# Second copies of keys and queries by SyncE's DMA queue in place of VectorE casts

## The reference

```
q_pool = q.reshape(B, H, S // 2, 2, D).mean(axis=3)          # 576 queries of 64
scores = scale * q_pool @ k.T ; scores -= max(scores)         # 576 x 1152
attn   = exp(scores) / (sum(exp(scores)) + 1e-9) ; out = attn @ v
x = out laid out as 2304 tokens x 512
h = x @ w_in ; x = (h * sigmoid(h)) @ w_out                   # 512 -> 2048 -> 512
out = ((x @ w1) * (x @ w2)) @ w3 @ w_out2                     # 512 -> 1024 -> 512
```

## Time and profile before

| | |
|---|---|
| median of 3 runs | 1469.06 us |
| span of the profiled execution, first to last instruction | 1465.5 us |
| mean granted clock of TensorE | 0.995 of full speed |
| busy: PE, DVE, ACT, POOL | 92%, 55%, 48%, 30% |
| DMA, hardware queue | 33648 packets, 75.73 MB, 19.1% of 16 engines |

### The profile page before, as it was taken

How to read it: one execution, slowest core, us unless ns; L and a number is a source line. 1 busy time by engine, 2 the same in 40 slices (tenths; PEclk the granted TensorE clock), 3 DMA queues, 4 the chain that set the end, 5 groups by cost and what they waited for, 6 DMA issues and landing times.

```text
span 1465.5 us, 24978 instructions
## 1 busy us (share of the span) xinstructions
PE 1352.9 (92%) x8224; PEld 1296.8 (88%) x8224; DVE 799.6 (55%) x1340; ACT 697.3 (48%) x1266; POOL 434.8 (30%) x322
## 2 busy tenths in 40 slices
PE   6888888888888888889999999999999999999998
PEld 5887877787778787778899999999999899999998
DVE  7888888888888889888531111111114522122221
ACT  4776666666666666667742222222224422121211
POOL 4766656666655766655200000000000000000000
PEclk9999999999999999999999999999999999999999
DMA  6233323333323233320220000000104200000000
GB/s 155 73 81 81 95 64 80 81 79 81 91 68 81 68 92 81 79 72 24 61 65 8 1 1 1 1 0 0 43 0 153 92 1 22 23 22 1 21 21 22
DMA packets 33694, 76.34 MB, mean 52 GB/s; under 512 B 8944, under 2 KB 12144, under 8 KB 33648
## 3 DMA queue, kind: packets, MB, share of 16 engines
q1 hardware_dynamic: 33648, 75.73, 19.1%
HBM read 70.84 MB, written 4.79 MB: 52 GB/s over the span
## 4 chain that ended last, share of the span: by engine, by line
PE 77%; DVE 13%; issue 7%; DVEq 1%; DMA 1%; ACT 0%; SPq 0%; ACTq 0%
PE psum L907 21%; PE psum L908 20%; PE psum L909 20%; PE psum L923 5%; PE psum L924 4%; DVE mx L708 4%; PE psum L948 3%; PE psum L949 3%; DVE mneg L717 2%; DVE pL L726 2%; DVE mneg L719 2%; PE psum L932 1%; DVE kB L691 1%; DVE xT L732 1%; DVE qHs L702 1%
## 5 line engine op out<-in xcount | busy, mean ns | idle before, releaser
L708 DVE TENSOR_REDUCE mx<-psum 128x1 f32<-128x384 f32 (+1 forms) x480 | 253.1, 548 | 74.3 <-PE psum L924 73.7
L516 ACT ACTIVATE pF<-psum 128x576 f32<-128x576 f32 x288 | 187.7, 652 | 158.9 <-PE psum L949 156.8
L923 PE MATMUL psum<-kA,qHm 128*128 128x384 f32 (+1 forms) x480 | 172.4, 359 | 60.5 <-DVE mx L708 50.4
L836 DVE TENSOR_TENSOR gL<-gF,gH 128x384 fp32r<-128x384 f32 x96 | 53.6, 558 | 306.0 <-ACT gH L593 306.0
L424 POOL TENSOR_TENSOR pL<-pF,pH 128x576 fp32r<-128x576 f32 x93 | 143.0, 1538 | 216.8 <-ACT pH L522 216.7
L522 ACT CAST pH<-pF 128x576 fp32r<-128x576 f32 x288 | 194.5, 675 | 4.6
L726 DVE TENSOR_TENSOR pL<-pF,pH 128x576 fp32r<-128x576 f32 x195 | 187.6, 962 | 15.0 <-ACT pH L522 14.5
L907 PE MATMUL psum<-pH,vH 128*128 128x288 f32 x576 | 178.7, 310 | 1.5 <-DVE xT L732 0.7
L590 ACT ACTIVATE gF<-psum 128x384 f32<-128x384 f32 x96 | 47.3, 492 | 261.9 <-PE psum L909 261.9
L909 PE MATMUL psum<-pH,vL 128*128 128x288 f32 x576 | 171.0, 297 | 0.0
L908 PE MATMUL psum<-pL,vH 128*128 128x288 f32 x576 | 170.8, 297 | 0.0
(11 more groups left out here) (88 smaller groups left out, 3030.0 us busy)
## 6 DMA issues: line engine op xcount, KB each, us to landing
qraw<-in_qT SPq DMA_DIRECT2D x64, 288.0 KB, 4.2
kraw<-in_kT SPq DMA_DIRECT2D x64, 288.0 KB, 5.1
vraw<-in_v SPq DMA_DIRECT2D x32, 288.0 KB, 2.7
rsums<-recips SPq DMA_DIRECT2D x32, 144.0 KB, 2.9
outT<-oS SPq DMA_DIRECT2D x6, 768.0 KB, 3.4
wstage<-in_w_in SPq DMA_DIRECT2D x16, 256.0 KB, 3.4
fstage<-in_w3T SPq DMA_DIRECT2D x8, 512.0 KB, 4.7
w12stage<-in_w SPq DMA_DIRECT2D x8, 512.0 KB, 4.7
```

The costliest lines, as they stand in the source:

```text
L516: act.activation(two(pF[r][:]), stbank[(NC * j + c) % 2], ACT.Exp, scale=SCALE).then_inc(exp_done, 1)
L708: dve.tensor_reduce(mx[0:m, qt, b:b + 1], max_bank(h, jj, t)[0:m, 0:KW], AX.X, ALU.max)\
L923: pe.matmul(out, qHm[jj][:, cols], kA[jj][:, kblock(b)], start=True, stop=False)
```

## The change

The kB, qBs and qHs copies are made by DMAs within SBUF, issued from SyncE, from the rounded kA, from qLm and from qHm (seen as plain fp32, so nothing is converted). Each buffer j has its own semaphore, counted by 16 a DMA; the waits of TensorE, GpSimd and ScalarE are on these. VectorE's three helpers and their calls go. SyncE's program for pairs 1 to 14 is written out instead of looped. In each head, the copies stand in SyncE's list at the places that the diff shows; load_k no longer waits for kB.

```
...
@@ -286,13 +286,23 @@

             def load_k(h, j):
                 need(sp, kA_lo, KB * (h - 1))
-                need(sp, kB_ready, KB * (h - 1))
                 for half in range(2):
                     sp.dma_start(kraw[j][D * half:D * half + D], kT[h]).then_inc(k_loaded[j], 16)

             def load_v(h):
                 need(sp, vL_ready, h)
                 sp.dma_start(vraw[:], v[h]).then_inc(v_loaded, 16)
+
+            def copy_k(h, j, b):
+                sp.wait_ge(kA_hi, KB * h + b + 1)
+                sp.dma_start(kB[j][0:D, kblock(b)].bitcast(F32), kA[j][0:D, kblock(b)].bitcast(F32)).then_inc(kB_copied[j], 16)
+
+            def copy_q(h, j):
+                need(sp, st_scored, NC * (h - 1))
+                sp.wait_ge(qLm_ready, h + 1)
+                sp.dma_start(qBs[j][0:D, :].bitcast(F32), qLm[j][0:D, :].bitcast(F32)).then_inc(qBs_copied[j], 16)
+                sp.wait_ge(qHm_ready, h + 1)
+                sp.dma_start(qHs[j][:].bitcast(F32), qHm[j][:].bitcast(F32)).then_inc(qHs_copied[j], 16)

             load_q(0)
             load_k(0, 0)
@@ -300,6 +310,11 @@
             load_k(1, 1)
             load_q(1)
             load_v(0)
+            copy_q(0, 0)
+            for b in range(KB):
+                copy_k(0, 0, b)
+            for b in range(KB):
+                copy_k(1, 1, b)

             def load_w(i):
                 need(sp, winL_ready, i)
@@ -317,8 +332,7 @@

             def spread_rsums(i):

-                at = i * P if isinstance(i, int) else sp.snap(i * P)
-                at2 = at + D if isinstance(i, int) else sp.snap(i * P + D)
+                at, at2 = i * P, i * P + D
                 sp.wait_ge(rpacked_ready, i + 1)
                 if isinstance(i, int) and i == PAIRS - 1:
                     sp.wait_ge(normalized, i)
@@ -333,20 +347,29 @@
                 first = isinstance(i, int) and i == 0
                 for j in range(2):
                     h = 2 * i + j
+                    more = not (last and j == 1)
+                    if more:
+                        copy_q(h + 1, 1 - j)
+                    if more and not (first and j == 0):
+                        copy_k(h + 1, 1 - j, KB - 1)
                     if not last:
                         load_q(h + 2)
                         load_k(h + 2, j)
-                    if not (last and j == 1):
+                    if more:
                         load_v(h + 1)
                     if j == 0:
                         load_w(i)
                         if not first:
                             pack_sums(i - 1)
-                if not first:
-                    spread_rsums(i - 1)
+                    if not last:
+                        copy_k(h + 2, j, 0)
+                    if j == 0 and not first:
+                        spread_rsums(i - 1)
+                    if not last:
+                        copy_k(h + 2, j, 1)

             pair(0, False)
-            with sp.Fori(1, PAIRS - 1) as i:
+            for i in range(1, PAIRS - 1):
                 pair(i, False)
             pair(PAIRS - 1, True)

@@ -398,7 +421,7 @@
                 pool.wait_ge(qHm_ready, h + 1)
                 pool.wait_ge(q_summed, h + 1)
                 need(pool, max_scored, ITEMS * (h - 1))
-                need(pool, qBs_ready, h - 1)
+                need(pool, qBs_copied[j], 8 * (h - j))
                 pool.tensor_tensor(qLm[j][:], qsum[:], qHm[j][:].bitcast(F32), ALU.subtract).then_inc(qLm_ready, 1)

             def k_lo(h, j, b, *before):
@@ -486,7 +509,7 @@
             def q_hi(h, j):
                 act.wait_ge(q_summed, h + 1)
                 need(act, max_scored, ITEMS * (h - 1))
-                need(act, qHs_ready, h - 1)
+                need(act, qHs_copied[j], 8 * (h - j))
                 act.copy(qHm[j][:], qsum[:]).then_inc(qHm_ready, 1)

             def k_hi(h, i, j, b):
@@ -577,7 +600,8 @@
                     act.copy(xH[e][:, k, :], xT[:, k, bass.ds(t * TILE, TILE)]).then_inc(ready, 1)

             act.wait_ge(kA_lo, KB * HEADS)
-            act.wait_ge(kB_ready, KB * HEADS)
+            for j in range(2):
+                act.wait_ge(kB_copied[j], 16 * KB * PAIRS)
             act.wait_ge(q_summed, HEADS)
             act.wait_ge(normalized, HPB)
             x_hi(0, 0, xH_ready, (h_ready, 0))
@@ -684,23 +708,6 @@
-            def k_b(h, i, j, b):
...
-            def q_b(h, j):
...
-            def q_hi_st(h, j):
...
@@ -749,18 +756,12 @@
                 dve.wait_ge(kA_hi, b + 1)
                 lo = kA[0][D:P, kblock(b)]
                 dve.tensor_tensor(lo, kraw[0][D:P, kblock(b)], lo.bitcast(F32), ALU.subtract).then_inc(kA_lo, 1)
-            q_b(0, 0)
-            q_hi_st(0, 0)
             for t in range(ITEMS):
                 take_max(0, 0, t)
                 if t == 2:
                     dve.wait_ge(ident_loaded, 16)
                     dve.tensor_copy(identR[:], ident[:]).then_inc(const_ready, 1)
-                if 3 <= t < 3 + KB:
-                    k_b(0, 0, 0, t - 3)
             negate_max(0)
-            for b in range(KB):
-                k_b(1, 0, 1, b)

             def pair(i, last):
                 first = isinstance(i, int) and i == 0
@@ -779,16 +780,6 @@
                         if more:
                             for t in items(s):
                                 take_max(h + 1, 1 - j, t)
-                        if s == 0 and more:
-                            q_b(h + 1, 1 - j)
-                        if s == 0 and more and not (first and j == 0):
-                            k_b(h + 1, i + j, 1 - j, KB - 1)
-                        if s == 3 and more:
-                            q_hi_st(h + 1, 1 - j)
-                        if s == 4 and not last:
-                            k_b(h + 2, i + 1, j, 0)
-                        if s == 7 and not last:
-                            k_b(h + 2, i + 1, j, 1)
                         if s == 6 and j == 0 and not first:
                             recip(i - 1)

@@ -933,13 +924,13 @@
                                         identR[0:m, 0:m])
                 last.then_inc(m_turned, 1)

-            def score_t(h, j, c):
+            def score_t(h, j, c, i):

                 if c == 0:
                     pe.wait_ge(m_placed, 2 * (h + 1))
-                    pe.wait_ge(qHs_ready, h + 1)
-                    pe.wait_ge(qBs_ready, h + 1)
-                    pe.wait_ge(kB_ready, KB * (h + 1))
+                    pe.wait_ge(qHs_copied[j], 16 * (i + 1))
+                    pe.wait_ge(qBs_copied[j], 16 * (i + 1))
+                    pe.wait_ge(kB_copied[j], 16 * KB * (i + 1))
                 need(pe, exp_done, NC * h + c - 1)
                 keys = slice(c * P, (c + 1) * P)
                 out = stbank[(NC * j + c) % 2]
@@ -981,7 +972,7 @@
                     h = 2 * i + j
                     more = not (last and j == 1)
                     for s in range(NC):
-                        score_t(h, j, s)
+                        score_t(h, j, s, i)
                         ahead = [(h + 1, 1 - j, t) for t in items(s)] if more else []

                         at_once = ahead if s in (LAG - 1, LAG) or (first and j == 0 and s < LAG) else ahead[:1]
```

More of the change, by code:

```diff
@@ L686, in _ @@
         def _(dve):
[L687 to L702, removed]
             def take_max(h, jj, t):
@@ L781, in pair @@
                                 take_max(h + 1, 1 - j, t)
[L782 to L791, removed]
                         if s == 6 and j == 0 and not first:
```

30 lines of the change are left out of this document (11 added, 19 removed).

## The result

| | before | after |
|---|---|---|
| median (range), us | 1469.01 (1468.89 to 1470.64) | 1598.17 (1587.10 to 1606.23) |
| span of the profiled execution | 1465.5 | 1593.3 |
| granted clock of TensorE, mean | 0.995 | 0.944 |

The change makes the kernel slower: ratio 1.0874, 95% interval 1.0849 to 1.0898, 129 us. The forecast was 1532, with a range up to 1572. The sign and the place were right, the size was half.

A forecast was written before the change was run, and what follows sets the result against it. TensorE bounds the kernel, held in attention by VectorE's maxima. Late loop +44, clock falls +29, earlier falls replaced -3, prologue -2, heads 0, 30, 31 -5: +63 on 1469 gives 1532 us, range 1485 to 1572.

The forecast's parts named there:

- SyncE's list loses its prefetch: SyncE's queue, heads 1 to 29: loads sit behind copies that wait for scores and ScalarE's rounding; +1.5 us a head.
- The copies hidden: Five SBUF copies a head on SyncE's queue: their own landing, even at 5.1 us, costs nothing.
- the late keys hidden: Key loads landing at 11.25 us make ScalarE wait some 2 us, hidden while TensorE is held until 13.6.
- the unrolling nothing: SyncE's program written out instead of looped costs nothing, since its issues lie hidden.
- T0: The moment at which TensorE starts the first transposed score of a head; 22.1 us a head before the change.
- The step that failed: the clock: TensorE's clock falls after the hole in about 26 of 29 heads, 1.1 us each: +29 us.
- The loop, short by the rest: Attention heads 1 to 29: late queries lengthen a head from 22.1 to 23.6 us, +44 us.
- the tail from values(h, 2) to the next T0: TensorE at the end of a head: 8.6 us of work plus 1.4 waiting for the negated maxima.
- Heads that I gave a gain: Heads 0, 30 and 31 keep their prefetch and lose the waits for the maxima: -5 us.
- The prologue: VectorE's casts between its first maxima go: -2 us.
- The rival that left the clock out: Late loads in attention while TensorE's clock holds: +37 us, 1506 us; chance 0.22.
- later still: Copy ahead of the query load delays its landing: 1.0 us a head, 29 us more, 1561 us; chance 0.16.

The follow-up runs named there:

- run with 20 needless matmuls: Changed kernel plus 20 needless TensorE matmuls (3.6 us) a head in step 4, ahead of tile 9 of the row maxima; 1549.07 us, ratio 1.0542.
- the run with the wait alone: Kernel before, all casts kept and no copies, plus SyncE's wait for ScalarE's rounding of the last key block ahead of each pass's loads; 1579.59 us, ratio 1.0760.
- fill 23: Changed kernel plus 23 needless TensorE matmuls (4.1 us) a head in step 4, ahead of tile 9 of the row maxima; 1552.35 us, ratio 1.0580.

## Why the prediction was wrong, step by step

**Right.** The bound and the place (TensorE waiting within attention, nothing after it). That SyncE's list loses its prefetch, for heads 1 to 29, by ScalarE's rounding in step 1. The copies hidden, the late keys hidden, the unrolling nothing. The start of the loop in the traced head: rounding ends at T0 + 3.9 (forecast 3.9), the second half of the queries is issued at 307.2, T0 + 5.0 (5.05), p_lo ends at 13.7 (13.55), a hole of 4.0 us (3 to 4).

**The step that failed: the clock.** I priced one fall in about 26 of 29 heads at 1.1 us, between the 0.9 of the one pair with a fall in the earlier trace rows and the 1.5 from the earlier trace rows: 29 us. Measured: 139 us at half clock in the 600 us that hold 22.6 heads, 6.2 us a head where one fall lasted 3.4. The clock's stretches show why. It fell in every one of the 29 heads with a hole, 14 to 18 us after the transposes of the negated maxima, in the hole or just behind it. Of the 23 such heads between 100 and 700 us, six had a fall of twice the length (the traced head is one, about 315.0 to 321.8). And in 12 heads the clock fell a second time, within 1 us after the stop for the negated maxima, where it had fallen 3 times before the change; that stop was 1.5 to 1.8 us in the 12 and 0.8 to 1.5 in the others.

Half of 6.2 is 3.1 us of work lost a head. What of it shows is the head of 26.5 less the heads without a fall, near 24.3: 2.2 us, 64 us over 29 heads, 35 more than my term. The run with 20 needless matmuls gives the same sum another way: 49 won, 6.4 paid in heads 0 and 30, and 0.3 us a head, 9 us, for the falls that it still has. What the prediction had wrong is above all the count: one stretch a head at most, where there were 1.8 (23 + 6 + 12 in 22.6 heads). The price of 1.1 was a little low. Against 24.3, from head 3 on, heads with one fall of 3.4 us took 25.6 to 26.1, those with the double one 25.9 to 26.2, those with two falls 26.6 to 27.5: 1.4 us for the first, 0.4 more where it lasts twice as long, 1.4 more for a second fall elsewhere.

**The loop, short by the rest.** 24.3 us in place of 23.6, so 64 us in place of 44. About half of the 0.7 lies in the chain to p_lo, and two errors partly cancel there, which was luck. The sum starts at 9.7 in the mean in place of 9.05. In the traced head the second half was issued on time and landed after 4.4 us; I had taken 4.0, the median of both halves, but the sum waits for the later one (4.2 for the pair of the earlier trace rows). GpSimd then took 4.2 us in that head, in place of 4.5, from the start of the sum to the end of p_lo: the sum and p_lo 1.40 each and the low keys 0.99, where my means were 1.61, 1.54 and 1.18. With all VectorE casts in place, in the run with the wait alone, the sum and p_lo take 1.4 too, so it isn't shown that the casts had stretched them.

The other half lies in the tail from values(h, 2) to the next T0, which I put at 8.6 of work and 1.4 of stop. In the second of my two heads I took off "about 1.4" for the stop for the negated maxima, where the row says 0.98:

```profile
324.38 0.52 PE L932 MATMUL psum<-identR,mneg 128*2 128x128 f32 x5 [0.98 <-DVE mneg L719]
```

So the work was 8.6 in one head and 9.0 in the other, 0.2 more in the mean than I took. The rest is p_lo(h, 5), which comes late by 0.5 us in the second head of a pair, where GpSimd's list has the weight slice and normalize before it. With fill 23 the tail takes 10.2 us in second heads and 10.4 to 10.5 in first ones. TensorE's timeline there, where the clock doesn't hide it, shows both waits of a second head:

```profile
310.70 0.40 PE L899 MATMUL psum<-pH,vH 128*128 128x288 f32 x1 [0.19 <-POOL pL L448]
...
317.21 0.40 PE L899 MATMUL psum<-pH,vH 128*128 128x288 f32 x1 [0.51 <-POOL pL L448]
```

**Heads that I gave a gain.** I took 5 us for heads 0, 30 and 31. Between the transposes, head 0 took 18.9 us for 19.1, the last 19.7 for 18.6: nothing. The prologue gained 1.7 us (2 forecast): the first transpose stands at 19.75 in place of 21.42 us.

The account in spans: 64 + 64 - 2 (prologue) + 1 (the last head) is 127 of 128 us. The split between loop and clock is good to some 5 us, since it rests on heads without a fall from kernels with a fill.

The rule of the Trainium skill's page "TensorE: Matmul & The Clock Gate", section "HAM oscillation — how this bites in real kernels", which the forecast weighed (a long enough wait for data in every iteration throttles the clock anew each time), held in its direction: all 29 heads with a hole, of 3.6 to 4.3 us, had a fall. It did not hold for every head in the other runs: with the wait alone four of 29 heads had none at holes of 3.0 us. The rival that left the clock out, 1506, would have been wrong by 92 us. The rival "later still" had the right direction for the landing, but put 1.0 us a head on it where the chain was 0.35 late.

## What to carry to other kernels

A DMA queue that one engine issues in order is a program: putting an operation with a late wait at its head moves every load behind it, and a prefetch of a whole head can vanish without a line of it being edited. For each added wait, list what is issued behind it and who is waiting for that; put loads that can start early ahead of copies that can't. Where a change opens a stop in every iteration of a loop that TensorE bounds, price the clock too: count the low stretches that one iteration can hold, and work out their price for the engine that stands on the loop. Where an operation waits for the later of two DMAs, take the landing of the later one.

## What the runs showed of the hardware

- A kernel with a stop of TensorE of about 2.4 us in every head spent as much time at half clock (140 us in 600) as one with 4.0 us (139), counting the falls behind its second stop of up to 1.8 us. With 1.5 us it was 17. A single stop does not decide it: heads with 3.0 us had no fall in the run with the wait alone (four), while the 1.8 us stop for the negated maxima brought one in 3 heads in the 600 us of the kernel before. Filling 2.7 us of idle time a head with needless matmuls won some 45 us (ratio 1.0566 against 1.0874).
- Copies within SBUF issued from SyncE landed in 2.0 us (64 x 384, 96 KB), 2.3 us (144 KB) and 2.5 us (288 KB), 0.46 to 0.60 us of issue each.
- The order of the list changed landing times too, without any copy: in the run with the wait alone a 2.2 KB DMA took 4.8 us (1.9 in the earlier trace rows) and the values load 5.5 (2.7 before), both issued shortly behind the late query and key loads. In the changed kernel they took 5.1 and 5.7.
- 24 MB more of such copies left the query loads at 4.1 us (4.2 before).
